# Three engines' orders in the rational layer of a fused attention and MoE kernel: where W4's conversions, the output subtractions and eight transposes stand

## The reference

```python
def _moe_ref(x, w_in, w_out, a, b):         # w_in 512 x 2048, w_out 2048 x 512
    h = x @ w_in
    h2 = h * h
    h3 = h2 * h
    P = a[0] + a[1] * h + a[2] * h2 + a[3] * h3
    Q = 1.0 + np.abs(b[0]) * np.abs(h) + np.abs(b[1]) * h2
    g = P / (Q + 1e-06)
    return (g @ w_out).astype(np.float32)

def _moe2_ref(x, w1, w2, w3, w_out):        # w1, w2, w3: 1024 columns, w_out 1024 x 512
    a = x @ w1
    b = x @ w2
    h = a * b @ w3
    return (h @ w_out).astype(np.float32)
```

## Time and profile before

| | |
|---|---|
| median of three runs | 811.91 us (811.78 to 812.69) |
| the profiled execution | 811.28 us, of which span 809.5 us |
| mean granted clock of TensorE | 0.987 of full speed |
| TensorE busy | 777.4 us (96%) |
| VectorE / ScalarE / GpSimd busy | 448.4 / 409.2 / 325.5 us |
| TensorE's waits on L487 (subtractions) | 1.2 us in 2 |
| TensorE's waits on L540 (rest of g), from 380 us | 4.1 us in 2 |
| one group of 12 matmuls (product_in or product_out) | 2.88 us |

### The profile page before, as it was taken

How to read it: one execution, slowest core, us unless ns; L and a number is a source line. 1 busy time by engine, 2 the same in 40 slices (tenths; PEclk the granted TensorE clock), 3 DMA queues, 4 the chain that set the end, 5 groups by cost and what they waited for, 6 DMA issues and landing times.

```text
span 809.5 us, 10852 instructions
## 1 busy us (share of the span) xinstructions
PE 777.4 (96%) x3761; PEld 607.1 (75%) x3761; DVE 448.4 (55%) x767; ACT 409.2 (51%) x662; POOL 325.5 (40%) x229
## 2 busy tenths in 40 slices
PE   5899999999998959999999998999999999999998
PEld 4677677677675638888788876887888888888886
DVE  6778888888885175667767776775441210110120
ACT  4266677677675466887766776774221011011101
POOL 0067677767766523674222213533332210210220
PEclk9799999999999989999999999999999999999999
DMA  8423423433421080200000002520200000001001
GB/s 201 113 60 92 107 70 88 105 81 89 98 71 30 20 228 2 72 1 1 0 1 1 0 1 104 204 108 27 79 0 1 1 26 27 1 14 39 0 0 52
DMA packets 51948, 44.80 MB, mean 55 GB/s; under 512 B 28577, under 2 KB 43201, under 8 KB 51905
## 3 DMA queue, kind: packets, MB, share of 16 engines
q1 hardware_dynamic: 49744, 41.29, 18.4%
q10 hardware_dynamic: 2160, 2.95, 1.2%
HBM read 28.35 MB, written 3.15 MB: 39 GB/s over the span
## 4 chain that ended last, share of the span: by engine, by line
PE 91%; DVE 3%; ACT 2%; POOL 1%; issue 1%; DMA 1%; SPq 0%; ACTq 0%; POOLq 0%
PE psum L813 87%; PE psum L818 3%; PE psum L601 1%; DVE psum L1277 1%; DMA RAWQK<-in_k 0%; ACT TT L394 0%; POOL PSUMS L1391 0%; DVE MROW L1277 0%; ACT P L1067 0%; DVE HH L460 0%; DVE TT L482 0%; POOL G L540 0%; DVE psum L478 0%; DVE TT L464 0%; DVE HH L474 0%
## 5 line engine op out<-in xcount | busy, mean ns | idle before, releaser
L813 PE MATMUL psum<-OPS 128*128 128x384 f32 x576 | 134.1, 362 | 7.9 <-DVE psum L1277 2.9
L1391 POOL TENSOR_TENSOR PSUMS<-PSUMS,P 128x768 f32<-128x768 f32 x64 | 117.3, 1832 | 39.4 <-ACT P L1067 39.3
L813 PE MATMUL psum<-XT,W 128*128 (+1 forms) x576 | 131.0, 389 | 0.0
L813 PEld LDWEIGHTS psum<-OPS 128*128 128x128 f32 x576 | 98.8, 194 | 39.9 <-issue 23.4
L540 POOL TENSOR_TENSOR G<-TT,G 128x512 fp32r<-128x512 f32 x48 | 62.3, 1297 | 164.8 <-ACT G L418 164.8
L813 PEld LDWEIGHTS psum<-XT,W 128*128 128x128 f32 x576 | 108.1, 188 | 22.5
L1067 ACT ACTIVATE P<-psum 128x768 f32<-128x768 f32 x96 | 77.6, 808 | 60.5 <-PE psum L813 57.7
L1277 DVE TENSOR_REDUCE psum<-psum 128x1 f32<-128x768 f32 x90 | 86.7, 963 | 35.4 <-PE psum L813 35.4
L715 DVE TENSOR_TENSOR ABF<-AS,psum 128x512 f32<-128x512 f32 x24 | 16.5, 687 | 146.8 <-ACT AS L689 146.8
L739 POOL TENSOR_TENSOR W<-ABF,W 128x512 fp32r<-128x512 f32 x24 | 30.9, 1289 | 147.2 <-DVE W L719 147.2
L813 PE MATMUL psum<-G,WSPLIT 128*128 128x512 f32 x360 | 86.6, 390 | 1.1 <-POOL G L540 1.1
(11 more groups left out here) (118 smaller groups left out, 1143.7 us busy)
## 6 DMA issues: line engine op xcount, KB each, us to landing
OPS<-OPS SPq DMA_DIRECT2D x32, 192.0 KB, 3.0
W3R<-in_moe_w SPq DMA_DIRECT2D x8, 512.0 KB, 3.3
W12RAW<-in_moe_w SPq DMA_DIRECT2D x8, 512.0 KB, 4.1
RAWQK<-in_q SPq DMA_DIRECT2D x16, 192.0 KB, 3.1
RAWQK<-in_k SPq DMA_DIRECT2D x16, 192.0 KB, 3.3
XT<-XH SPq DMA_DIRECT2D x32, 96.0 KB, 2.2
XT<-XL SPq DMA_DIRECT2D x32, 96.0 KB, 2.1
out<-OS SPq DMA_DIRECT2D x12, 256.0 KB, 2.0
```

The lines of the kernel that those rows point to most:

```text
L813: return nc.tensor.matmul(o, stationary, moving, start=start, stop=stop, skip_group_check=True)
L1391: nc.gpsimd.tensor_tensor(total, P32[:, (2 * u[1]) % 4, :] if n == 1 else total, P32[:, (2 * u[1] + n) % 4, :], ALU.add).then_inc(p_added, 1)
```

## The change

Three places in the engines' orders change. No instruction is added or removed, apart from semaphore waits.

- TensorE: the two calls of `transpose_w3` in the last loop are written behind product_out(n) at n = 45, where they stood ahead of product_out(n) at n = 46.
- ScalarE and GpSimd: W4_AT goes from 36 to 38, so W4's eight conversions and their rests stand in bodies 38 to 45 and not 36 to 43. The wait ahead of the first, for out_done at 36, becomes one for 35, and a wait for 36 comes ahead of the fifth.
- VectorE: the four output subtractions of chunks 0 and 1 stand behind `cubic(n)`, ahead of newton_second(n - 1), cubic_end(n) and quotient(n - 1), where they stood behind those.

```diff
             for n in range(LAST - LAG, LAST):
-                if n == LAST - LAG + 1:
-
+                product_out(n)
+                if n == LAST - LAG:
                     transpose_w3(0)
                     transpose_w3(1)
-                product_out(n)
@@ def split_w4_hi(i)
                 act.wait_ge(ld_w4, 16)
-                if i == 0:
-                    act.wait_ge(out_done, 2 * NF + 4)
+                if i % 4 == 0:
+                    act.wait_ge(out_done, 2 * NF + 3 + i // 4)
                 nc.scalar.copy(W4[:, 1, i, :], W4RAW[:, 0, i, :]).then_inc(w4_hi, 1)
@@ rational_vector
                 cubic(dve, n)
+                if n % NF == 2 and n > NF:
+                    y_rest(n // NF - 1)
                 newton_second(n - 1)
                 cubic_end(dve, n)
                 quotient(n - 1)
                 if 1 <= n <= 3:
                     divide((3, 3), n - 1)
-                if n % NF == 2 and n > NF:
-                    y_rest(n // NF - 1)
@@
-        W4_AT = 2 * NF + 4
+        W4_AT = 2 * NF + 6
```

## The result

The changed kernel took 805.71 us (median of 6, 804.51 to 807.26), the kernel before 812.61 us (median of 6, 811.78 to 814.38): a ratio of 0.9915, 95% interval 0.9899 to 0.9930. That is 6.9 us less, with an interval of 5.7 to 8.2. Forecast were 4.95 us less and a time of 806.96 us, in a range that reached down to 806.0. The profiled execution took 805.25 us, with a span of 803.4.

The account below looks back on a forecast made before the run. TensorE, busy 777.4 of 809.5 us, was taken to bound the kernel, so only its stalls could be won back. Gains of 0.86, 0.85 and 3.24 us summed to 4.95, giving 806.96 us, range 806.0 to 808.7.

Parts of the forecast that it names:

- Part 1: TensorE's transposes near output product 45: same instruction list and waits, so 0.00 us, bounded by -0.4 and 0.
- Part 2: Output subtractions at both chunk ends: moving them removes TensorE's excess of 0.86 and 0.85 us, 1.71 us gained.
- Rival A: Late quotients cause a new wait ahead of output products 17 and 33, cancelling Part 2; 808.67 us, chance 0.07.
- Part 3: W4's conversions: later place and earlier condition end ScalarE's block and TensorE's stall before output product 36; 3.24 us gained, 2.72 at worst.
- The sum: Whole kernel: 0.86 + 0.85 + 3.24 = 4.95 us gained, 806.33 for the profiled execution, 806.96 for the median.
- B: TensorE's stalls: only their idle time, 4.16 us, comes back and the 0.79 us of restart stays; 807.75 us, chance 0.03.
- C: Rounds 38 to 45: W4's conversions bring another stall of the old size, only Part 2 counts; 810.20 us, chance 0.03.
- D: Behind the rational stage: a late load or split at the folds gives the gain back; 811.9 us, chance 0.02.
- E: Chunk ends: VectorE and ScalarE fall into lockstep, two lost rounds at each boundary make it slower; 817.8 us, chance 0.02.

Follow-up runs that it names:

- e1: Only TensorE's hunk of the change (the transpose calls, same instruction list) made to the kernel before; 812.39 us, ratio 0.9992.
- e2: Only the four output subtractions moved, against the kernel before; 812.51 us, ratio 0.9994.
- e3: Only W4's conversions moved to bodies 38 to 45 with both their waits, against the kernel before; 808.66 us, ratio 0.9940.
- e4: The whole change run once more, against the kernel before; 805.02 us, ratio 0.9913.
- e7: The whole change plus the eight transposes put ahead of output product 45; 807.55 us, ratio 0.9930 to the kernel before.
- e8: The whole change plus 16 transposes of the identity at the very start; 804.30 us, ratio 0.9883 to the kernel before.
- e5: The kernel before plus 12 matmuls by zeros ahead of TensorE's 3 us wait before output product 36; 813.25 us, ratio 0.9993.
- e10: The whole change with e9's six ScalarE waits, plus 12 matmuls by zeros on TensorE at each place; 824.46 us, ratio 1.0144 to the kernel before.
- e9: The whole change plus ScalarE waits for out_done at n ending bodies 20, 24, 28, 36, 40, 44; 828.94 us, ratio 1.0202 to the kernel before.
- e11: As e9, on the whole change, with a longer ScalarE block (h_ready, n + 4); 851.86 us, ratio 1.0494 to the kernel before.
- e12: As e9, on the whole change, with a shorter ScalarE block (h_ready, n + 3); 808.25 us, ratio 0.9942 to the kernel before.
- e13: The kernel before, unchanged, profiled again, first of four looks; profiled execution 812.73 us, in(16) to first fold 189.57 us.
- e16: The kernel before, unchanged, profiled again, last of four looks; profiled execution 812.13 us, in(16) to first fold 191.19 us.
- e6: The whole change but W4's conversions kept in bodies 36 to 43 with the new waits; 807.19 us, ratio 0.9924 to the kernel before.

## Why the prediction was wrong

Point by point:

- Part 1, the transposes, 0.00: right. e1's interval holds 1, and the order after is that of before.
- Part 2, the subtractions, 1.71: right, with its inner times. Subtractions 0.62 us behind the copies, newton_second 2.40 us on, round_g 0.06 us later than before relative to the copies. Rival A's wait appears in no profile. The median of e2 doesn't show the gain (0.5 us less, from 1.9 less to 0.9 more); the stage does.
- Part 3, W4, 3.24: the mechanism is right, the size is not. This is the mis-sized term. The spacing in the profile was worth 3.15 (e3) to 3.24, and e3's median came 4.9 us under before (3.1 to 6.7). I had summed the term from one execution, in which the clock was 1.00 throughout the stage, and took that for the kernel. Behind a wait of 2.96 us the clock falls in some executions and not in others, and the wait then costs up to 6.1 us. That execution was a lucky one for the kernel before: three of the seven profiles had no fall, four had one. Averaged over the seven the term is 3.24 + 1.3 = 4.5, and the sum 6.2 us, inside the measured 5.7 to 8.2. My bounds for the part, 2.72 and 3.24, had only a loss in them: nothing above the value that I took.
- The sum, and the range's lower end: the step "so 806.33 for it; the median ... is 0.63 higher, and gives 806.96" took the gain from one profile and the time from a median of three. Over six runs that median is 812.61, 0.70 higher; so the time missed by 1.25 us only, the gain by 1.95. The kernel before had further medians of 812.68, 813.82 and 812.66. Three runs within 0.9 us were too few to take the scatter from.
- Rivals B, C, D and E: the rest after the fold is 249.3 to 249.4 us in every profile, against D; there is no wait in the W4 rounds, against C; the restart went with its stall, against B; both rounds at the chunk ends are 5.44 us and none is lost behind them, against E.

What stays open is the 0.7 us between 6.2 and 6.9, and how much of the 1.3 the medians hold. Four kernels whose stages are alike to 0.14 us (the change, e4, e7, e8) came out 6.9, 7.1, 5.7 and 9.5 us under before, so 0.7 is less than such comparisons differ by. And 1.08 of the 6.10 us between the spans of the first two profiles lies ahead of in(16). That start scattered from 368.57 (e4) to 372.79 us (e1) over the fifteen profiles without e5, e8 and e10, which have instructions of their own there. The six of them that hold the whole change (after, e4, e7, e9, e11, e12) average 370.4 us, from 368.57 to 371.52, and the other nine 371.6. No instruction differs there, so scatter is the likely reading, and not shown to be all of it.

The mean clock of whole executions doesn't settle the 1.3 either. A loss of 1.3 us takes 2.6 us at half clock, 0.0016 of the mean. Over 78 executions with the 3 us wait (before, e1, e2, e13 to e16) it averages 0.9862, over 48 without it (after, e3 to e7, e12) 0.9863, with an error of 0.0007 on the difference. That doesn't bear out so large a share; but nearly all of the time at half clock lies ahead of in(16), it scatters there by more than what is sought, and part of the start can read 1.00 wrongly (last section). So it is shown that the clock falls behind the wait in some executions, and that part 3 had no term for it. That this makes up the gap in the medians is likely and not shown.

## What to carry to other kernels

A stall of TensorE is worth its idle time, its restart and, behind the waits of 2.38 us and more measured here, a chance of matmuls at half clock (behind those up to 1.11 us there was none, and none between was measured): look behind every such wait for groups that are longer than their like, in more than one profile, before summing. One profile of a kernel is one draw; cut traces at two events that enclose the change, and the stage tells 0.1 us apart where medians of whole executions don't tell 1.5. And when a moved wait frees one engine, ask which of the two, the looser condition or the later place, does the work: here the condition gave most of it (e6).

## What the runs showed that was not expected

The clock's answer to a stall is not the same from one execution to the next. Waits of 2.38 us in one execution had a fall behind them or none, behind 2.95 us the loss was 0, 1.7 or 2.8 us, 5.08 to 5.61 us always had one, and waits up to 1.11 us in that stage never did. The start of an execution varies too. TensorE's first 12 small matmuls took 2.71 us in the profile before and 1.48 in the one after, both with 1.00 in the clock column for the stretch from 8 to 12 us (before, then after):

```profile
10.39 2.71 PE L813 MATMUL psum<-CT,OPS 128*128 128x32 f32 x12 [1.00 <-DVE OPS L1189]
```

```profile
10.40 1.48 PE L812 MATMUL psum<-CT,OPS 128*128 128x32 f32 x12 [1.08 <-DVE OPS L1188]
```

That the longer one ran at half clock can be read from e8, whose column has a low level there, where the same group took 2.61 us. Behind it the same kind of work has the same pace in both kernels, with 0.50 in the one column and 1.00 in the other (e8, then before; the clock is the third figure from the end):

```profile
10.00:22.00 12.00, 10.02 (x45) 9.55 (x46) 9.43 (x20) 4.26 (x7) 0.00 (x0) 0.50 1.08 290
```

```profile
12.00:24.00 12.00, 10.01 (x44) 9.44 (x43) 8.62 (x20) 4.85 (x7) 0.00 (x0) 1.00 1.09 297
```

So a clock column of 1.00 near the start is not to be relied on; the length of like groups is.

A third draw lies ahead of in(16): TensorE's wait for the last of the attention's output rows to be placed (XT<-XL) was 0.3 us in the profile after and 1.7 in e3, with the same instructions up to there.
